# First batch of a fused attention and mixer kernel: half of x^T comes by scratch memory and VectorE's 32x32 transposes, and one half-batch of q, k and alpha is loaded later

## The chip, the core and the metric

The kernel runs on one core of one Trainium2 chip. The metric is the device time of one execution in microseconds; lower is better. TensorE (PE) multiplies matrices, VectorE (DVE), ScalarE (ACT) and GpSimd (POOL) work on elements, and SyncE (SP) issues nearly all DMAs. All engines run their own instruction streams and meet only at semaphores.

## The reference, cut to what matters

A gated linear attention over 4 batches, 8 heads, 768 tokens and head size 48 gives x; a token mixer and a channel mixer follow, and a last gated feed-forward layer.

```python
# attention, per batch and head
state = alpha[t][:, None] * state + outer(k[t], v[t])
y[t] = q[t] @ state                                  # x = y of all heads: (768 tokens, 384)
# token mixer and channel mixer
xt = x.transpose(0, 2, 1)
h = np.maximum(xt @ w_tok1, 0.0) @ w_tok2
u = x + h.transpose(0, 2, 1)
x2 = u + np.maximum(u @ w_ch1, 0.0) @ w_ch2
# gated feed-forward on x2 and its shifted copy (w_k, w_v, w_r)
```

The line that the change touches is `u = x + h^T`. The kernel keeps u with the 384 features on partitions, so it needs x^T, while the attention leaves x with the tokens on partitions.

## The kernel before

**Stages.** The program is one hand-written order for each engine. First comes the attention of batch 0 (the "head", `head_part`), in 24 steps: step i is token chunk c = i // 4 (128 tokens) and head pair p = i % 4. The loop runs over slots s = 0 to 27; in slot s the transposes and decay scans of step s run beside the scores of step s-2 and the outputs of step s-3. Then, for r = 1 to 3, the attention of batch r runs beside the mixer of batch r-1 (`batch_slot`, 28 slots each), then the mixer of batch 3 alone, then the feed-forward layer. From the end of the head on PE has matmuls of the mixer in every slot.

**Head, engine by engine.** In slot s ACT first copies the output of step s-3 out of PSUM (`high_x`: L953 to `x_sum`, L954 to `x_hi`), then spreads q of step s (`spread_q`, L975, semaphore `qbd_ready`), and then rounds half of one weight piece to `hi` (`split_half_hi`, L920): piece n is done in slots 3 + 2n and 4 + 2n, so piece 9 in slots 21 and 22. DVE does in each slot `mask`, `scans` (L1137, L1139), `scale_qk` (L1146 to L1154) and `outputs` (L1187, which waits for `xhi_ready` of step s-3). PE's scores of step i (L669, slot i+2) wait for `qbd_ready` of step i. POOL makes `x_lo` (`low_x`, semaphore `xlo_ready`) and the low part of each weight piece (semaphore `w_lo_ready`).

**Weights.** w_tok1, w_tok2, w_ch1 and w_ch2 are cut into 16 pieces of 384 KB, loaded one after the other into a ring of three buffers `w_raw`; pieces 0 to 9 are split in the head, piece 9 being the last of w_ch1; 10 to 15 are w_ch2. SP issues piece n once POOL has finished piece n-3. The slots in which SP comes to them: piece 9 in slot 16, piece 10 in 18, 11 in 20, 12 in 22.

**q, k, alpha and v of later batches.** `load_half(r, n)` loads 384 tokens of a head pair of batch r in 12 small DMAs (L367), `load_half_v(r, n)` the v beside them in 2 (L381). They fill `qka0`/`vt0` for even n and `qka1`/`vt1` for odd n. Steps 0 to 2 of batch 1 read half-batch (1, 0), steps 3 to 5 half-batch (1, 1); DVE's `turn` (L1124) of step 3 is in slot 4 of `batch_slot(1, ...)`.

**x^T.** For batches 1 to 3 x goes out to scratch memory (`store_x`), comes back in 32-row blocks (`load_x_blocks`, 4 DMAs for 128 features and 384 tokens) and is transposed by DVE in 32x32 blocks (`turn_x`, L1266); `down_base` then adds it to the token mixer's output (L1280). For batch 0 PE itself transposes x out of `x_sum` into the PSUM bank in which the token mixer's second product is then summed up (`token_down`, L767, `is_transpose`), and `down_base` only copies (L1275).

**After the head.** DVE does `split_low(1, 0)` (L1164, the low part of q of batch 1, step 0) and `tile_first(0, 0)`/`tile_second` (L1245, `h_lo`). PE claims a bank of `b_ring` for each tile of `token_down`, the first when `h_lo` has been read out of it (`tile_lo`). Token half 0 is tiles m = 0 to 2, half 1 the next three.

Of the kernel before, what the change touches and what calls it, by code (L numbers as in the profile page):

```python
# [13 lines left out]
def attention_mixer_channel_mix(nc, q, k, v, alpha, w_tok1, w_tok2, w_ch1, w_ch2,  # L14
# [39 lines left out]
    with ctx:  # L54
# [158 lines left out]
        x_raw_loaded = [sem(f"x_raw_loaded{n}") for n in range(2 * KC)]  # L213
        x_turned = sem("x_turned")
        x2_stored = [sem(f"x2_stored{n}") for n in range(2)]
        x2_loaded = [sem(f"x2_loaded{n}") for n in range(2)]
# [122 lines left out]
        def _(sp):  # L339
# [50 lines left out]
            def load_x_blocks(b, k):  # L390

                sp.wait_ge(x_rows_stored, 16 * (2 * KC * (b - 1) + k + 1))
                for a in range(4):
                    sp.dma_start(x_sum[32 * a:32 * (a + 1), k, :].rearrange("p (n j) -> p n j", j=32),
                                 x_rows[b][k].rearrange("(n p) (a j) -> a p n j", p=32, j=32)[a])\
                      .then_inc(x_raw_loaded[k], 16)

            def load_piece(n):
                dst, loaded, _ = staging(n)
# [21 lines left out]
            for s in range(SLOTS):  # L421

                if s % NP == 0 and 0 < s < NP * (NC - 2):
                    load_qka(s // NP + 2)
                if s % NP == 3 and 3 < s < NP * (NC - 2):
                    load_v(s // NP + 2)
                if s % NP == 0 and s >= NP * (NC - 2) and s < STEPS:
                    load_half(1, s // NP - NC + 2)
                if s % NP == 3 and s >= NP * (NC - 2) and s < STEPS:
                    load_half_v(1, s // NP - NC + 2)  # L430
                for n in pieces_in(s):
                    load_piece(n + NRAW)
            for n in range(2, 5):
                if n == 2:
# [195 lines left out]
        def _(pe):  # L630
# [131 lines left out]
            def token_down(b, half, m):  # L762
                t = KT + KC * half + m
                dst = claim(b, t)
                if b == 0:
                    for n in range(TM):
                        nc.tensor.matmul(dst[:, n * P:(n + 1) * P], x_sum[:, TM * half + n, m * P:(m + 1) * P],  # L767
                                         ident[:, :], start=(n == 0), stop=False, is_transpose=True)
                for n in range(3 * KT):
                    kt, (i, j) = n // 3, PASSES[n % 3]  # L770
                    if t == KT:
                        if i == 0:
                            pe.wait_ge(tile_hi, TILES * b + kt + 1)
                        else:
                            pe.wait_ge(tile_lo, TILES * b + kt + 3)
                    mm = nc.tensor.matmul(dst, h1[i][:, kt, m * P:(m + 1) * P], tok2_w(j, kt, half),  # L776
                                          start=(b > 0 and n == 0), stop=(n == 3 * KT - 1))
                mm.then_inc(tile_done, 1)
# [327 lines left out]
        def _(dve):  # L1106
# [143 lines left out]
            def read_sums(b, half):  # L1250

                for m in range(KC):
# [3 lines left out]
                                            ALU.add).then_inc(acc_read, 1)  # L1256

            def turn_x(b, k):

# [8 lines left out]
            def down_base(b, n):  # L1268
# [4 lines left out]
                dve.wait_ge(tile_done, TILES * b + t + 1)  # L1273
                if b == 0:
                    ins = nc.vector.tensor_copy(x2_half[half][:, m, :], src)  # L1275
# [56 lines left out]
            for s in range(SLOTS):  # L1332
                head_part(s)
            dve.wait_ge(mu_loaded, 32)
            nc.vector.tensor_scalar(omu[:, :, :], mu[:, :, :], -1.0, 1.0, ALU.mult, ALU.add).then_inc(omu_ready, 1)
# [74 lines left out]
```

## Time and profile before

| | |
|---|---|
| median of 3 runs | 732.37 us (732.33 to 732.41) |
| the profiled execution, its own time | 732.72 us |
| its span, first to last instruction | 731.0 us |
| PE busy | 725.3 us (99% of the span) |
| DVE busy | 472.0 us (65%) |
| ACT busy | 331.0 us (45%) |
| POOL busy | 197.1 us (27%) |
| granted clock of PE | 1.00 |

Times in the trace are counted from the start of the span. Some 1.7 us of an execution lie outside of the span. The clock of PE is granted in full in all 40 slices of the page. A busy share is an average over the whole program: the head, which ends at some 54 us, is limited by other things than the 670 us behind it.

### The profile page before, as it was taken

To read this page: it belongs to the slowest core of one execution; us is meant where nothing else is said; L and a number is where in the kernel's file an instruction comes from. 1 tells how busy PE (TensorE), PEld (TensorE's weight loads), DVE (VectorE), ACT (ScalarE), POOL (GpSimd) and SP (SyncE) were. 2 spreads that over 40 slices of the span, in tenths; PEclk is the share of its full clock that TensorE was granted. 3 is DMA by queue.
4 is the path that set the end of the run, shared out by engine and by line. 5 is a ranking of instruction groups with operands and counts; after the bars stand their busy time and mean duration, and the time that the engine had idled before them with its cause. 6 is when DMAs were issued, how large, how long until landed. Compare 5 with 4: busy or idle time off the path is not lost.

```text
span 731.0 us, 13851 instructions
## 1 busy us (share of the span) xinstructions
PE 725.3 (99%) x4556; PEld 719.3 (98%) x4556; DVE 472.0 (65%) x1297; ACT 331.0 (45%) x953; POOL 197.1 (27%) x344
## 2 busy tenths in 40 slices
PE   8999999999999999999999999999999999999998
PEld 8999999999999999999999999999999999999998
DVE  6988888865888875888883412446457375473561
ACT  4866544432544442444442332436346264373550
POOL 3875564333243331334432440310000000000000
PEclk9999999999999999999999999999999999999999
DMA  9973545542425544343531224010011010110000
GB/s 205 219 153 75 95 58 108 83 74 64 57 41 86 104 81 76 51 55 56 111 62 33 87 86 141 33 33 34 33 53 44 33 38 28 53 43 32 11 22 32
DMA packets 210043, 50.90 MB, mean 70 GB/s; under 512 B 190400, under 2 KB 207168, under 8 KB 209984
## 3 DMA queue, kind: packets, MB, share of 16 engines
q1 hardware_dynamic: 206992, 45.11, 31.1%
q0 software_dynamic: 1152, 4.72, 1.7%
q8 instruction: 29, 0.48, 0.3%
q10 hardware_dynamic: 1840, 0.34, 0.2%
q14 instruction: 30, 0.25, 0.1%
HBM read 37.17 MB, written 12.98 MB: 69 GB/s over the span
## 4 chain that ended last, share of the span: by engine, by line
PE 98%; DMA 1%; DVE 0%; issue 0%; ACT 0%; SPq 0%; DVEq 0%
PE bank L788 21%; PE bank L804 21%; PE bank L884 14%; PE bank L862 14%; PE bank L706 5%; PE bank L871 5%; PE bank L674 4%; PE bank L776 3%; PE bank L745 3%; PE bank L711 2%; PE bank L704 2%; PE bank L669 2%; PE bank L646 1%; PE bank L757 1%; PE bank L682 1%; PE bank L828 1%
## 5 line engine op out<-in xcount | busy, mean ns | idle before, releaser
L981 ACT ACTIVATE hid_hi<-bank 128x384 fp32r<-128x384 f32 x96 | 47.2, 492 | 115.5 <-PE bank L788 115.2
L1245 DVE SCALAR_TENSOR_TENSOR hid_lo<-bank,hid_hi 128x384 fp32r<-128x384 f32 x96 | 53.2, 555 | 65.5 <-ACT hid_hi L981 64.5
L1081 ACT ACTIVATE relu_k<-bank 128x384 f32<-128x384 f32 x64 | 31.5, 491 | 106.0 <-PE bank L862 86.2
L788 PE MATMUL bank<-u_hi,wch_hi 128*128 128x384 f32 x288 | 72.1, 358 | 0.0
L788 PE MATMUL bank<-u_lo,wch_hi 128*128 128x384 f32 x288 | 66.3, 338 | 0.0
L804 PE MATMUL bank<-hid_lo,wch_hi 128*128 128x384 f32 x288 | 65.5, 334 | 0.0
L788 PE MATMUL bank<-u_hi,wch_lo 128*128 128x384 f32 x288 | 65.5, 334 | 0.0
L804 PE MATMUL bank<-hid_hi,wch_hi 128*128 128x384 f32 x288 | 65.4, 334 | 0.0
L804 PE MATMUL bank<-hid_hi,wch_lo 128*128 128x384 f32 x288 | 65.4, 334 | 0.0
L1377 DVE TENSOR_TENSOR x_half<-bank,x_half 128x384 f32<-128x384 f32 x24 | 13.4, 558 | 77.4 <-PE bank L884 75.3
L557 POOL TENSOR_SCALAR_AFFINE_SELECT relu_k<-relu_k 128x256 f32<-128x256 f32 x72 | 29.3, 407 | 112.3 <-ACT relu_k L963 112.2
L954 ACT ACTIVATE x_hi<-bank 128x96 fp32r<-128x96 f32 x96 | 23.5, 245 | 78.1 <-PE bank L711 65.4
L1164 DVE SCALAR_TENSOR_TENSOR qs_lo<-qkd,rhead,qs_hi 96x128 fp32r<-96x128 f32 x144 | 50.8, 392 | 10.1 <-ACT qs_hi L975 9.3
L1363 DVE TENSOR_TENSOR relu_k<-relu_k 128x384 f32<-128x384 f32 x64 | 35.7, 558 | 27.8 <-ACT relu_k L1081 24.8
L788 PEld LDWEIGHTS bank<-u_lo,wch_hi 128*128 128x128 f32 x288 | 52.1, 188 | 0.0
L788 PEld LDWEIGHTS bank<-u_hi,wch_lo 128*128 128x128 f32 x288 | 51.5, 188 | 0.0
L804 PEld LDWEIGHTS bank<-hid_hi,wch_hi 128*128 128x128 f32 x288 | 51.2, 188 | 0.1
L804 PEld LDWEIGHTS bank<-hid_hi,wch_lo 128*128 128x128 f32 x288 | 51.3, 188 | 0.0
L804 PEld LDWEIGHTS bank<-hid_lo,wch_hi 128*128 128x128 f32 x288 | 51.3, 188 | 0.0
L562 POOL TENSOR_TENSOR ks_lo<-qkd,ks_hi 96x128 fp32r<-96x128 f32 x72 | 32.9, 457 | 62.5 <-ACT ks_hi L971 61.3
L706 PE MATMUL bank<-vt,relu_k 128*128 128x48 f32 x352 | 49.7, 264 | 0.0
L975 ACT ACTIVATE qs_hi<-qkd,rhead 96x128 fp32r<-96x128 f32 x144 | 49.0, 388 | 0.0
(141 smaller groups left out, 1833.6 us busy)
## 6 DMA issues: line engine op xcount, KB each, us to landing
w_raw<-in_moe_w_ch SPq DMA_DIRECT2D x12, 384.0 KB, 3.6
x_scratch<-x_half POOLq DMA_DIRECT2D x8, 576.0 KB, 3.6
out<-x_half SPq DMA_DIRECT2D x24, 192.0 KB, 1.9
vt<-in_v SPq DMA_DIRECT2D x48, 72.0 KB, 2.3
x_scratch<-x_sum SPq DMA_DIRECT2D x18, 192.0 KB, 2.1
x_sum<-x_scratch SPq DMA_DIRECT2D x72, 48.0 KB, 2.2
qka<-in_q SPq DMA_DIRECT2D x49, 48.0 KB, 2.2
qka<-in_alpha SPq DMA_DIRECT2D x49, 48.0 KB, 2.2
```

Source lines behind the costliest of these rows:

```text
L562: nc.gpsimd.tensor_tensor(ks[1][0:W2, i % 2, :], qkd[0:W2, second_of(i), :], ks[0][0:W2, i % 2, :], ALU.subtract)\
L706: mm = nc.tensor.matmul(y_ps[:, h * D:(h + 1) * D], am[:, i % 2, h * P:(h + 1) * P], v_of(r, i)[:, h * D:(h + 1) * D], start=(h == 0 and c ...
L788: mm = nc.tensor.matmul(dst, ch1_w(a, n % KC, jj), u[c][:, n % KC, half * HT:(half + 1) * HT], start=(n == 0), stop=(n == 3 * KC - 1))
L804: mm = nc.tensor.matmul(b_acc[m][:, 0:HT], ch2_w(a, jj, m), hid[c][:, j % HJ, :], start=(jj == 0 and n == 0), stop=(jj == NJ - 1 and n == 2))
L862: mm = nc.tensor.matmul(dst, wk_w(a, n % KC, j), mix_out[0][c][:, n % KC, :], start=(n == 0), stop=(n == 3 * KC - 1))
L871: mm = nc.tensor.matmul(b_acc[m][:, 0:DM], mix_out[1][a][:, n % KC, m * P:(m + 1) * P], wr_w(c, n % KC), start=(n == 0), stop=(n == 3 * KC ...
L884: mm = nc.tensor.matmul(bank[m][:, 0:DM], k2[a][:, n % NF, m * P:(m + 1) * P], wv_w(c, n % NF), start=(n == 0), stop=(n == 3 * NF - 1))
L975: nc.scalar.activation(dst[0:W2, h * P:(h + 1) * P], qkd[0:W2, first_of(i), :], ACT.Copy, scale=rhead[0:W2, i % 4, h:h + 1])\
L981: nc.scalar.activation(dst, b_ring[t % 2][:, 0:HT], func).then_inc(tile_hi, 1)
L1164: nc.vector.scalar_tensor_tensor(qs[1][0:W2, i % 2, cols], qkd[0:W2, first_of(i), :], rhead[0:W2, i % 4, h:h + 1], qs[0][0:W2, i % 2, cols ...
L1245: ins = nc.vector.scalar_tensor_tensor(dst, src, 0.0, hi, ALU.max, ALU.subtract)
L1363: nc.vector.tensor_tensor(relu_k[:, j % 2, :], relu_k[:, j % 2, :], relu_k[:, j % 2, :], ALU.mult).then_inc(k2_ready, 1)
```

## The change

For token half 0 of batch 0 (tokens 0 to 383) the way of the later batches is taken. SP stores these rows of `x_sum` to scratch memory in three DMAs (`store_first_x`, in slot 16, behind `load_half(1, 0)`), waits until they have landed and loads them back into `x_sum` in 12 DMAs (`load_first_x_blocks`, in slot 19, behind `load_half_v(1, 0)`). DVE transposes them into `x2_half[0]` in slots 25, 26 and 27 of the head (`turn_first_x`), and `down_base` adds that to the bank. PE's nine transposes of this half are gone; those of half 1 stay. `load_half(1, 1)` and `load_half_v(1, 1)`, which stood in slots 20 and 23, come after SP's loop over the slots.

```diff
+            def store_first_x():
+                sp.wait_ge(xlo_ready, NP * TM)
+                for m in range(KC):
+                    sp.dma_start(x_rows[0][m].rearrange("(c p) f -> p c f", p=P),
+                                 x_sum[:, 0:TM, m * P:(m + 1) * P]).then_inc(first_rows_stored, 16)
+
+            def load_first_x_blocks():
+                sp.wait_ge(first_rows_stored, 16 * KC)
+                for m in range(KC):
+                    for a in range(4):
+                        sp.dma_start(x_sum[32 * a:32 * (a + 1), m, :].rearrange("p (n j) -> p n j", j=32),
+                                     x_rows[0][m].rearrange("(n p) (a j) -> a p n j", p=32, j=32)[a])\
+                          .then_inc(first_raw_loaded[m], 16)
...
-                if s % NP == 0 and s >= NP * (NC - 2) and s < STEPS:
-                    load_half(1, s // NP - NC + 2)
-                if s % NP == 3 and s >= NP * (NC - 2) and s < STEPS:
-                    load_half_v(1, s // NP - NC + 2)
+                if s == NP * (NC - 2):
+                    load_half(1, 0)
+                    store_first_x()
+                if s == NP * (NC - 2) + 3:
+                    load_half_v(1, 0)
+                    load_first_x_blocks()
                 for n in pieces_in(s):
                     load_piece(n + NRAW)
+            load_half(1, 1)
+            load_half_v(1, 1)
...
-                if b == 0:
+                turned_by_pe = b == 0 and half == 1
+                if turned_by_pe:
                     for n in range(TM):
                         nc.tensor.matmul(dst[:, n * P:(n + 1) * P], x_sum[:, TM * half + n, m * P:(m + 1) * P],
                                          ident[:, :], start=(n == 0), stop=False, is_transpose=True)
...
+            def turn_first_x(m):
+                dve.wait_ge(first_raw_loaded[m], 64)
+                nc.vector.transpose(x2_half[0][:, m, :], x_sum[:, m, :]).then_inc(first_turned, 1)
...
-                if b == 0:
+                if b == 0 and half == 0:
+                    dve.wait_ge(first_turned, m + 1)
+                    ins = nc.vector.tensor_tensor(x2_half[0][:, m, :], src, x2_half[0][:, m, :], ALU.add)
+                elif b == 0:
                     ins = nc.vector.tensor_copy(x2_half[half][:, m, :], src)
...
             for s in range(SLOTS):
                 head_part(s)
+                if STEPS + 1 <= s <= STEPS + KC:
+                    turn_first_x(s - STEPS - 1)
```

SP's stream from the end of `load_half(1, 0)` (slot 16) on, before. `qka0` is the buffer of half-batch (1, 0), `qka1` that of (1, 1), `w_ch1` is piece 9, the `w_ch2` rows are pieces 10, 11, 12 and 13:

```order
L367 DMA qka0<-in_alpha 32x12x32
L404 DMA w_raw<-in_moe_w_ch1 128x768
L404 DMA w_raw<-in_moe_w_ch2 128x2x384
L381 DMA vt0<-in_v 128x3x48 x2
L367 DMA qka1<-in_q 32x12x32
...
L367 DMA qka1<-in_alpha 32x12x32
L404 DMA w_raw<-in_moe_w_ch2 128x2x384 x2
L381 DMA vt1<-in_v 128x3x48 x2
L404 DMA w_raw<-in_moe_w_ch2 128x2x384
```

The same place of the changed kernel (its own line numbers):

```order
L370 DMA qka0<-in_alpha 32x12x32
L405 DMA x2_scratch<-x_sum 128x3x128 x3
L422 DMA w_raw<-in_moe_w_ch1 128x768
L422 DMA w_raw<-in_moe_w_ch2 128x2x384
L384 DMA vt0<-in_v 128x3x48 x2
L412 DMA x_sum<-x2_scratch 32x12x32 x12
L422 DMA w_raw<-in_moe_w_ch2 128x2x384 x2
L370 DMA qka1<-in_q 32x12x32
...
L370 DMA qka1<-in_alpha 32x12x32
L384 DMA vt1<-in_v 128x3x48 x2
L422 DMA w_raw<-in_moe_w_ch2 128x2x384
```

Three stores now stand ahead of piece 9, and twelve block loads take the place of the twelve loads of half-batch (1, 1), which come behind pieces 11 and 12.

DVE's stream at the end of the head and the start of batch 1, of the changed kernel, from the last instruction of `scale_qk(1, 0)` on:

```order
L1177 TENSOR_TENSOR qkd<-bank,decays 96x2x128 [waits scores_done,suffix_ready]
L1284 STREAM_TRANSPOSE x_half<-x_sum 128x384 [waits first_raw_loaded0]
L1284 STREAM_TRANSPOSE x_half<-x_sum 128x384 [waits first_raw_loaded1]
L1284 STREAM_TRANSPOSE x_half<-x_sum 128x384 [waits first_raw_loaded2]
L1368 TENSOR_SCALAR omu<-mu 128x6 [waits mu_loaded]
L1187 SCALAR_TENSOR_TENSOR qs_lo<-qkd,rhead,qs_hi 96x128 [waits qbd_ready,rhead_ready]
L1187 SCALAR_TENSOR_TENSOR qs_lo<-qkd,rhead,qs_hi 96x128 [waits qbd_ready]
L1268 SCALAR_TENSOR_TENSOR h_lo<-bank,h_hi 128x384 [waits tile_hi] x2
```

The three transposes are new; the other rows stood one behind the other before. `split_low(1, 0)` and `h_lo` are now queued behind the last of the twelve block loads.

## Rows read from the trace of the kernel before

**Rows 1.** The page, busy time of each engine.

```profile
PE 725.3 (99%) x4556; PEld 719.3 (98%) x4556; DVE 472.0 (65%) x1297; ACT 331.0 (45%) x953; POOL 197.1 (27%) x344
```

**Rows 2.** ACT in order of time, 45.5 to 48.3 us; in brackets idle time before.

```profile
46.31 0.53 ACT L920 ACTIVATE wch_hi<-w_raw 128x384 fp32r<-128x384 f32 x1 [0.37 <-DMA w_raw<-in_moe_w_ch]
...
46.87 0.24 ACT L954 ACTIVATE x_hi<-bank 128x96 fp32r<-128x96 f32 x1
47.08 0.69 ACT L975 ACTIVATE x_half<-qkd,rhead 96x128 f32<-96x128 f32 x2
```

**Rows 3.** DVE in order of time, 46 to 49 us.

```profile
47.15 0.31 DVE L1187 SCALAR_TENSOR_TENSOR state<-state,decays,bank 96x96 f32<-96x96 f32 x1
```

**Rows 4.** PE in order of time, 46 to 49 us: start, us, engine, line, work.

```profile
47.92 0.67 PE L669 MATMUL bank<-x_half,qkd 96*128 96x256 f32 x2
```

**Rows 5.** SP's DMA issues in order of time, 24 to 80 us.

```profile
40.70 2.30 SPq L367 DMA_DIRECT2D qka<-in_alpha  x4
43.04 0.94 SPq L404 DMA_DIRECT2D w_raw<-in_moe_w_ch  x2
44.03 1.00 SPq L381 DMA_DIRECT2D vt<-in_v  x2
45.08 2.10 SPq L367 DMA_DIRECT2D qka<-in_q  x4
...
52.13 0.98 SPq L404 DMA_DIRECT2D w_raw<-in_moe_w_ch  x2
```

**Rows 6.** PE in order of time, 56 to 64 us.

```profile
56.10 0.52 PE L767 MATMUL bank<-ident,x_sum 128*128 128x128 f32 x3 [0.29 <-DVE h_lo L1245]
...
59.51 0.49 PE L767 MATMUL bank<-ident,x_sum 128*128 128x128 f32 x3
...
62.29 0.28 PE L674 MATMUL bank<-qs_hi,ks_hi 96*128 96x256 f32 x1
```

**Rows 7.** PE in order of time, 177 to 180 us, token mixer of batch 1.

```profile
177.64 0.42 PE L776 MATMUL bank<-wtok_hi,h_hi 128*128 128x384 f32 x1
...
179.81 0.28 PE L674 MATMUL bank<-qs_hi,ks_hi 96*128 96x256 f32 x1
```

**Rows 8.** Line L767, PE's transposes.

```profile
L767 PE MATMUL bank<-ident,x_sum x18: 270/272/300, 56.1 to 64.3; 128*128 128x128 f32 x18
```

**Rows 9.** Lines L1275 and L1280, down_base.

```profile
L1275 DVE COPY x_half<-bank x6: 557/557/558, 57.7 to 65.7; 128x384 f32<-128x384 f32 x6
...
L1280 DVE TENSOR_TENSOR x_half<-bank,x_half x9: 520/558/559, 176.3 to 412.5; 128x384 f32<-128x384 f32 x9
```

**Rows 10.** Line L1266, DVE's transposes of x of later batches.

```profile
L1266 DVE STREAM_TRANSPOSE x_half<-x_sum x9: 567/568/570, 128.3 to 410.0; 128x384 f32<-128x384 f32 x9
```

**Rows 11.** DVE in order of time, 51 to 68 us.

```profile
51.53 0.41 DVE L1154 TENSOR_TENSOR qkd<-bank,decays 96x256 f32<-96x256 f32 x1
...
54.10 0.71 DVE L1164 SCALAR_TENSOR_TENSOR qs_lo<-qkd,rhead,qs_hi 96x128 fp32r<-96x128 f32 x2 [2.08 <-ACT qs_hi L975]
55.40 1.09 DVE L1245 SCALAR_TENSOR_TENSOR h_lo<-bank,h_hi 128x384 fp32r<-128x384 f32 x2 [0.59 <-ACT h_hi L981]
...
67.05 0.58 DVE L1124 STREAM_TRANSPOSE bank<-qka 96x384 f32<-96x384 f32 x1
```

**Rows 12.** Line L387, the stores of x of later batches.

```profile
L387 SPq DMA_DIRECT2D x_scratch<-x_sum x18: 383/384/432, 102.3 to 399.6; - x18
```

**Rows 13.** DMAs issued from 43.0 to 43.4 us: KB each, us to landing.

```profile
w_raw<-in_moe_w_ch SPq DMA_DIRECT2D x1, 384.0 KB, 3.2
```

**Rows 14.** Windows: PE, PEld, DVE, ACT, POOL busy, PE's clock, DMA share, GB/s.

```profile
103.00:104.00 1.00, 1.00 (x9) 1.00 (x9) 1.00 (x3) 0.64 (x3) 0.65 (x2) 1.00 0.79 212
```

**Rows 15.** Line L912, ACT's splits of pieces 10 to 12.

```profile
L912 ACT ACTIVATE wch_hi<-w_raw x3: 829/838/849, 56.3 to 68.5; 128x768 fp32r<-128x768 f32 x3
```

**Rows 16.** The page, DMA issues: KB each, median us to landing.

```profile
x_scratch<-x_sum SPq DMA_DIRECT2D x18, 192.0 KB, 2.1
x_sum<-x_scratch SPq DMA_DIRECT2D x72, 48.0 KB, 2.2
```

More of the change, by code:

```diff
@@ L214, in attention_mixer_channel_mix @@
         x_turned = sem("x_turned")
+        first_rows_stored = sem("first_rows_stored")
+        first_raw_loaded = [sem(f"first_raw_loaded{n}") for n in range(KC)]
+        first_turned = sem("first_turned")
         x2_stored = [sem(f"x2_stored{n}") for n in range(2)]
@@ L776, in token_down @@
                     mm = nc.tensor.matmul(dst, h1[i][:, kt, m * P:(m + 1) * P], tok2_w(j, kt, half),
-                                          start=(b > 0 and n == 0), stop=(n == 3 * KT - 1))
+                                          start=(n == 0 and not turned_by_pe), stop=(n == 3 * KT - 1))
                 mm.then_inc(tile_done, 1)
```

## The prediction, on record before the changed kernel ran

> **What bounds the kernel now.** I read the page first: PE is busy for 725.3 of 731.0 us [rows 1], so whatever PE loses or wins between the head and the end stays in the time; no later stage has an idle PE that could absorb it. The head is the exception: there PE, DVE and ACT pass the same step around, so I read it in order of time at 46 to 49 us, where the change puts its DMAs. ACT splits the first half of weight piece 9 at 46.31, after 0.37 us of waiting for its DMA [rows 2]: already now this piece comes late. DVE's state update L1187 at 47.15 [rows 3] comes right behind the copy `x_hi` that ACT finishes at 46.87 + 0.24 = 47.11 [rows 2]. PE's scores at 47.92 [rows 4] come right behind `spread_q`, finished at 47.08 + 0.69 = 47.77 [rows 2]. In this place ACT thus has no slack towards either of them. SP is the third thing to see: it issues without a break from 40.70 on, about 0.5 us for each DMA, and so it is late against its slots [rows 5]. Piece 9 is issued at 43.04 because that is when SP gets there.
>
> **Removed: nine transposes of PE.** Two tiles with transposes take from 59.51 to 62.29, 2.78 us [rows 6]; two tiles of batch 1 without them, from 177.64 to 179.81, 2.17 us [rows 7]. So a tile gets 0.305 us cheaper, and three **0.9 us**. A transposing instruction is listed with 272 ns [rows 8], but it overlaps its neighbours; 9 x 0.272 = 2.45 us is the upper end, nothing (if PE then waited for a bank) the lower. I take 0.9, because the difference of two pitches counts what the queue sees. PE has no wait inside these tiles behind the first one, at 56.10 [rows 6].
>
> The Trainium skill, "TensorE: Matmul & The Clock Gate", Part 4, gives about 275 ns for a PE transpose in a kernel's context. The rows agree with this as a duration (272 ns), not as a pitch; by that rule the change would win 2.5 us here in place of 0.9. That is rival 3 below.
>
> **Added on DVE: three block transposes and an add for a copy.** The add from PSUM takes 558 ns, as the copy does with 557 [rows 9]: nothing. The transposes take 0.57 us each [rows 10]. Their place is behind `scale_qk(1, 0)`, which ends at 51.53 + 0.41 = 51.94; DVE then idles 2.08 us until 54.10 [rows 11], which holds all three, 1.7 us. They cost nothing unless their blocks are late, which is the second wait below; without this cover they would cost up to 1.7.
>
> **Added on SP, the first wait: piece 9.** The three stores stand ahead of piece 9. The wait in front of them, for `xlo_ready` of step 11 (slot 14), is over: ACT is in slot 21 at 46.31 [rows 2]. Issue takes 0.384 us each [rows 12] and some 0.05 between, together 1.3 us, so piece 9 is issued at 44.35 in place of 43.04. It landed 3.2 us after its issue [rows 13]; with nothing else this gives a delay of 1.3, the lower end. But the stores also bring 3 x 196.6 = 590 kB. A stretch with such a store moved 212 GB/s with 0.79 of the DMA engines busy [rows 14], so 268 GB/s when full: 590 kB take 2.2 us. If the piece waits for all of it, the delay is 2.2. With issue stalls on a full queue (the twelve DMAs from 45.08 to 52.13 took 7.05 us, where 12 x 0.515 = 6.2 would do [rows 5]) I put the upper end at 2.6. I take **1.9**, nearer the full transfer, since the stores' bytes go first.
>
> "DMA: Bandwidth & Descriptors", Queues, rings and completion order, in the Trainium skill says that each DMA engine consumes the descriptors of a ring in order. No row here shows two such DMAs apart; by that rule alone the delay would be 2.2.
>
> What is queued behind: ACT waits at the split of piece 9 in slot 21, and `x_hi` of step 19 and `spread_q` of step 22 stand behind it. DVE's L1187 and PE's L669 follow directly, so the head from 46.3 on moves by the same 1.9. Neither can work ahead: DVE's next mask and scans stand behind L1187, PE's outputs and token products behind L669. From 48 us on PE has no idle time in which to make it up. Pieces 10 to 12 are also later, but ACT splits them from 56.3 to 68.5 only [rows 15].
>
> **Added on SP, the second wait: the blocks.** The last store is issued at about 43.9. One lands after 2.1 us alone [rows 16]; three in a row should land by 46.9. SP meanwhile issues two pieces (0.98) and v (1.00) [rows 5] and is there at 46.4. The twelve block loads take 6.2 to 7.05 us, so the last is issued at 52.6 to 53.5 and lands 2.2 later [rows 16], at 54.8 to 55.7; call it T, 55.3. DVE then needs 0.57 for the last transpose, the small `omu` and 0.71 for `split_low`, so `h_lo` can begin at T + 1.3 = 56.6. Before it began at 55.40 [rows 11]; with the head moved by 1.9 it is due at 57.3. So the second wait is hidden behind the first by some 0.7 us and adds nothing. Were the first gone, it would cost 56.6 - 55.4 = 1.2 by itself. The two don't add up: PE loses the larger.
>
> **Moved: half-batch (1, 1).** Twelve loads and two of v go past twelve block loads and pieces 11 and 12. After the blocks (53.1 to 54.0) and the pieces (0.98) they start at 54.1 to 55.0, take up to 7.05 and land by 64.3. DVE's `turn` of step 3 reads them at 67.05 [rows 11], about 1 us later with the shift. At least 2.7 us are left: nothing. Pieces 11 and 12, issued now at 52.13 [rows 5], come 1 to 2 us later, and ACT comes to them long behind piece 10: nothing. Piece 13 waits for POOL anyway.
>
> **Sum.** +1.9 (piece 9) + 0 (blocks, hidden) - 0.9 (transposes) = +1.0 us on a span of 731.0, so 732.0; with the 1.7 us outside of it the profiled execution would take 733.7, against 732.72 before. The median of the runs is 0.35 lower than that execution: 732.37 + 1.0 = 733.4.
>
> **The rivals.** A measurement of this kernel can tell about 0.2% from no change, 1.46 us, so bounds are 730.9 and 733.8.
>
> Forecast, chance 0.68: delays of 1.3 to 2.6 for piece 9, less 0.9, is +0.4 to +1.7: 732.8 to 734.1. About a third of it is over 733.8.
>
> Rival 1, slower, 0.12: the blocks are late after all. SP would have to lose 2 us more, as when one issue takes over 1.7 us because the DMA queue is full (the stores, two pieces and v are about 1.5 MB within 3 us), or the stores' landing is late. It decides once T is later than 56.0; at T = 57.4, PE loses 3.3 and wins 0.9: +2.4, 734.8. For it speaks the stretch from 45.08, 0.9 us slower than its issue pitch; against it that this 0.9 is already in my 53.5.
>
> Rival 2, no change, 0.08: piece 9 is not held up, since stores and loads overlap and its landing was long only because of its neighbours. Then the blocks alone cost 1.2: +0.3, 732.7.
>
> Rival 3, a little faster, 0.05: the transposes give back their whole 2.45 us. 1.9 - 2.45 = -0.55: 731.8.
>
> Rival 4, faster, 0.07: neither wait reaches PE, since the head has slack that I don't see. -0.9 gives 731.5, and with the full price of the transposes -2.45, 729.9; about half of it passes the bound.
>
> **How the numbers follow.** The predicted time is the forecast's, 733.4. The range has to reach from rivals 2 to 1; 731.9 to 735.0 leaves out rivals 3 and 4 and the late end of rival 1, together under 2 in 10. Slower by over 0.2%: 0.22 of the forecast and all of rival 1, 0.34. Faster: 0.06 from rivals 3 and 4. The rest, 0.60, is within 0.2%.
>
> **What would show it.** In the profile after: three stores of x from about 43.0 and piece 9 at 44.3; ACT idle about 2.2 us before a split L-line of `wch_hi`, released by the DMA into `w_raw`, where 0.37 stood; PE idle for about 1.9 us before its scores at some 49.8. The three block transposes of DVE around 54 to 56, the last with a wait for its DMA, and no wait of `split_low` that names them. The first token product about 1.9 us later than 56.1, and three tiles of 1.1 us in place of 1.4. SP's loads for `qka1` from about 54.5, with no wait for them at DVE's `turn`. The step most likely wrong is the delay of piece 9: if ACT's wait there is under 1.3 or over 2.6, my DMA argument fails. If PE idles for a second time before its first token product, it is the blocks.

## The result: 0.65% slower, 5.5 us where 1.0 was forecast

| | before | changed |
|---|---|---|
| median | 732.43 us (732.33 to 732.94, 6 runs) | 737.94 us (736.05 to 739.61, 6 runs) |
| the profiled execution | 732.72 us | 737.68 us |
| its span | 731.0 us | 736.0 us |
| mean granted clock, each run | 1.0 | 0.998; 0.995 three times; 0.993 twice |

The ratio is 1.0065 with a 95% interval of 1.0038 to 1.0091: slower, and above the predicted range of 731.9 to 735.0. The runs of the changed kernel spread over 3.6 us where those of before spread over 0.6, and they go with the clock: 736.05 at 0.998, three at 737.6 to 738.2 and 0.995, the two above 739 at 0.993. The two medians alone would give a ratio of 1.0075. Each experiment below has its ratio to the kernel before on its own chip.

The page of the changed kernel, engines and granted clock:

```profile
PE 727.7 (99%) x4547; PEld 721.5 (98%) x4547; DVE 473.1 (64%) x1300; ACT 331.0 (45%) x953; POOL 197.2 (27%) x344
...
PEclk9998999999999999999999999999999999999999
```

PE has nine instructions fewer and is nevertheless 2.4 us longer busy than in [rows 1]. The fourth slice of the clock, from 55 us on, is lower than the others. Busy time that grows while work shrinks is the first sign that a wait is not all that was added.

**The first wait.** A DMA is issued when SP hands it over, and lands when its data is there and its semaphore says so. SP's stream in the timeline (start, duration to the last of a group, line, count):

```profile
42.42 1.56 SPq L405 DMA_DIRECT2D x_scratch<-x_sum  x3
44.02 1.22 SPq L422 DMA_DIRECT2D w_raw<-in_moe_w_ch  x2
45.29 1.05 SPq L384 DMA_DIRECT2D vt<-in_v  x2
46.68 7.41 SPq L412 DMA_DIRECT2D x_sum<-x_scratch  x12
54.13 0.98 SPq L422 DMA_DIRECT2D w_raw<-in_moe_w_ch  x2
55.16 1.99 SPq L370 DMA_DIRECT2D qka<-in_q  x4
```

Piece 9 is issued at 44.02. The head runs 0.35 us ahead of the execution of before in this one, so against the work around it the issue is 0.98 + 0.35 = 1.33 us later than the 43.04 of [rows 5]. That is the 1.3 worked out, with some luck: the three stores took 1.60 us of SP, and the alpha loads ahead of them 0.30 less than before (2.00 for 2.30). How long it took to land, from the DMA view of 44.0 to 44.5 us (last column: us from issue to landing):

```profile
w_raw<-in_moe_w_ch SPq DMA_DIRECT2D x1, 384.0 KB, 5.1
```

It was 3.2 us in [rows 13]. To the start of ACT's split it is 5.08 now and was 3.27. ACT in the timeline:

```profile
49.10 0.52 ACT L943 ACTIVATE wch_hi<-w_raw 128x384 fp32r<-128x384 f32 x1 [3.51 <-DMA w_raw<-in_moe_w_ch]
...
49.66 0.24 ACT L977 ACTIVATE x_hi<-bank 128x96 fp32r<-128x96 f32 x1
49.80 0.68 ACT L998 ACTIVATE x_half<-qkd,rhead 96x128 f32<-96x128 f32 x2
```

Where ACT waited 0.37 us in [rows 2] it waits 3.51: 3.14 more, 1.33 of it from the issue and 1.81 from the landing. `x_hi` and `spread_q` follow at once, as they did before. PE's timeline shows the gap, and three places by which to measure what is behind it:

```profile
50.62 0.67 PE L691 MATMUL bank<-x_half,qkd 96*128 96x256 f32 x2 [2.99 <-DVE relu_k L1194]
...
60.97 0.28 PE L696 MATMUL bank<-qs_hi,ks_hi 96*128 96x256 f32 x1
...
61.83 0.41 PE L799 MATMUL bank<-wtok_hi,h_hi 128*128 128x384 f32 x1 [0.26 <-issue]
...
70.26 0.36 PE L726 MATMUL bank<-state,qkd 96*128 96x96 f32 x2
```

The first are the scores that stood at 47.92 [rows 4]: +2.70. The second are the scores of batch 1, step 0; the last the first state product of batch 1 behind the tiles of the token mixer. The two in the kernel before:

```profile
55.21 0.28 PE L674 MATMUL bank<-qs_hi,ks_hi 96*128 96x256 f32 x1
...
65.48 0.36 PE L704 MATMUL bank<-state,qkd 96*128 96x96 f32 x2
```

From the first place to the second it is 7.29 us before and 10.35 now: **3.06 us more, with not one instruction more and no new wait of that size**. From the second to the third it is 10.27 before and 9.29 now: the transposes give back 0.98. 2.70 + 3.06 - 0.98 = 4.8 of the 5.0 by which the spans differ.

**The clock.** The busy times by windows of 2 us tell where the 3.06 are:

```profile
core 0: us, PE busy (x) PEld busy (x) DVE busy (x) ACT busy (x) POOL busy (x), PEclk, DMA share, GB/s
...
48.00:50.00 2.00, 0.00 (x0) 0.00 (x0) 0.06 (x1) 0.90 (x4) 0.02 (x1) 1.00 0.89 182
50.00:52.00 2.00, 1.38 (x10) 1.35 (x11) 1.96 (x8) 1.26 (x6) 1.74 (x3) 1.00 0.50 80
52.00:54.00 2.00, 2.00 (x8) 1.91 (x7) 1.44 (x4) 0.86 (x4) 1.49 (x3) 0.56 0.57 92
54.00:56.00 2.00, 2.00 (x9) 1.91 (x9) 1.46 (x6) 0.39 (x2) 0.00 (x0) 0.50 0.70 116
56.00:58.00 2.00, 2.00 (x10) 2.00 (x8) 1.04 (x4) 0.00 (x0) 0.39 (x1) 0.50 0.99 340
58.00:60.00 2.00, 2.00 (x11) 2.00 (x11) 0.24 (x1) 1.17 (x5) 0.75 (x2) 0.73 0.96 121
60.00:62.00 2.00, 1.74 (x12) 1.57 (x11) 1.30 (x4) 1.32 (x4) 0.07 (x1) 1.00 0.58 70
```

PE stands still through 48 to 50, resumes at full clock, and from 52 on is granted 0.50, that is 1.2 GHz in place of 2.4. In "2.00 busy" it now completes 8 to 11 instructions, and the others wait for it. One minus the granted clock, times 2 us, summed over the rows, estimates the time that the clock took: 0.88 + 1.00 + 1.00 + 0.54 = 3.4 us. I call this the clock's share below. It is a little too high, since the two places above are only 3.06 us further apart.

**The blocks.** DVE in the timeline:

```profile
55.50 1.48 DVE L1284 STREAM_TRANSPOSE x_half<-x_sum 128x384 f32<-128x384 f32 x3
...
59.76 0.72 DVE L1187 SCALAR_TENSOR_TENSOR qs_lo<-qkd,rhead,qs_hi 96x128 fp32r<-96x128 f32 x2 [2.72 <-ACT qs_hi L998]
```

The three transposes run without a wait (the last block was issued at 53.62 and landed 2.0 us later, at 55.6), and `split_low` behind them waits for ACT, not for a block. The slow clock had a part in that: DVE came to them late, behind a wait of 1.04 us (at 54.51) for PE's slowed scores.

### The profile page after: what moved, and what is told of

It reads as the page before. It is cut to its first block, busy times and chain, and to the rows that moved or that the text cites. A ratio compares the mean times of both kernels' runs of the same rounds, so it can differ in the third digit from the quotient of the medians.

```text
span 736.0 us, 13854 instructions
## 1 busy us (share of the span) xinstructions
PE 727.7 (99%) x4547; PEld 721.5 (98%) x4547; DVE 473.1 (64%) x1300; ACT 331.0 (45%) x953; POOL 197.2 (27%) x344
## 4 chain that ended last, share of the span: by engine, by line
PE 93%; DVE 4%; DMA 1%; issue 1%; POOL 0%; ACT 0%; SPq 0%; DVEq 0%; POOLq 0%
PE bank L811 21%; PE bank L827 20%; PE bank L907 14%; PE bank L885 14%; PE bank L894 5%; PE bank L728 4%; PE bank L696 4%; PE bank L799 3%; PE bank L767 3%; PE bank L726 2%; PE bank L733 2%; DVE relu_k L1194 1%; PE bank L779 1%; DVE decays L1160 1%; DVE decays L1162 1%
## 5 line engine op out<-in xcount | busy, mean ns | idle before, releaser
L1187 DVE SCALAR_TENSOR_TENSOR qs_lo<-qkd,rhead,qs_hi 96x128 fp32r<-96x128 f32 x144 | 51.0, 393 | 10.6 <-ACT qs_hi L998 9.7
```

What stands on the lines that cost most here:

```text
L1187: nc.vector.scalar_tensor_tensor(qs[1][0:W2, i % 2, cols], qkd[0:W2, first_of(i), :], rhead[0:W2, i % 4, h:h + 1], qs[0][0:W2, i % 2, cols ...
```

## The experiments

The theory after the result: piece 9 is held up by the sum of issue and bytes, and the gap that this opens in PE's stream brings the clock down. The rival within it: the clock falls for another reason (the blocks, the new order, the slower DVE), and would fall without the gap. The other rival: it is the wait for the blocks that costs.

### The stores alone, and with an eighth of their bytes

`stores only` is the kernel before with the three stores and SP's wait for their landing; `small stores` writes 16 of the 128 partitions. Nothing else of the change is in them.

```diff
+                if s == NP * (NC - 2):
+                    store_first_x()
                 if s % NP == 3 and s >= NP * (NC - 2) and s < STEPS:
                     load_half_v(1, s // NP - NC + 2)
+                if s == NP * (NC - 2) + 3:
+                    sp.wait_ge(first_rows_stored, 16 * KC)
...
+                    sp.dma_start(x_rows[0][m].rearrange("(c p) f -> p c f", p=P)[0:16],   # small stores
+                                 x_sum[0:16, 0:TM, m * P:(m + 1) * P]).then_inc(first_rows_stored, 16)
```

> The kernel before with nothing but the three stores of x ahead of weight piece 9 (and the wait for their landing in slot 19). The output is the reference's; no block loads, no block transposes, PE keeps all its transposes. Theory A (the stores hold up piece 9, ACT waits, PE's gap lets the clock fall): ACT waits about 3.5 us for the piece, PE idles about 3 us at 47.5, the granted clock is 0.5 to 0.6 for some 6 us behind it, and the time is that of the changed kernel plus the 0.9 us of the transposes, 737 to 740. Rival B (the blocks or the moved half-batch do the damage): 732 to 733.5 with a clock of 1.00.

> As e1_stores_only, but each store takes 16 of the 128 partitions, an eighth of the bytes (only that part of scratch memory is written, and nothing reads it). If the bytes hold up piece 9: it lands about 1 us later than before (issue time of three DMAs), ACT waits about 1.3 us, no fall of the clock, 733 to 734. If it is the number of DMAs in the queue whatever their size: as e1, ACT waits 3 us or more.

Measured: stores only 738.94 us (737.06 to 741.13, 7 runs), ratio 1.0076 [1.0054, 1.0098]; small stores 737.65 (733.57 to 741.22, 10 runs), 1.0046 [1.0015, 1.0078]. ACT in the timeline of stores only, and then of small stores:

```profile
49.89 0.52 ACT L931 ACTIVATE wch_hi<-w_raw 128x384 fp32r<-128x384 f32 x1 [4.10 <-DMA w_raw<-in_moe_w_ch]
```

```profile
48.35 0.52 ACT L931 ACTIVATE wch_hi<-w_raw 128x384 fp32r<-128x384 f32 x1 [2.83 <-DMA w_raw<-in_moe_w_ch]
```

Three stores do it all; x^T, the blocks and the moved half-batch are not needed for the loss. The piece was issued at the same time in both (44.35 and 44.37) and ACT's split began 5.54 and 3.98 us later: seven eighths of the bytes are about 1.6 us, in one profiled execution each. So the bytes count on top of the issue. But I expected small stores at 733 to 734 with a wait of 1.3, and it missed: ACT waited 2.46 us more than before. Against the work around it the piece was issued 1.75 us late, not 1.0, and it landed 0.7 us more slowly than in the kernel before. PE's row in small stores, and the window of 48 to 50 us:

```profile
49.87 1.19 PE L680 MATMUL bank<-x_half,qkd 96*128 96x256 f32 x2 [2.31 <-DVE relu_k L1182]
```

```profile
48.00:50.00 2.00, 0.13 (x1) 0.16 (x1) 0.81 (x3) 1.65 (x6) 0.73 (x2) 0.82 1.02 259
```

A gap of 2.31 us, and the clock took 3.4. Here it had fallen before PE came back: the window has 0.82 although PE stood still for nearly all of it, and the first scores take 1.19 us where 0.67 is usual.

### The gap filled with idle products

The changed kernel, with 16 products of the identity that nobody reads ahead of PE's slot 24. The kernel before already has such products (`keep_warm`) in its first slots.

```diff
             for s in range(SLOTS):
+                if s == STEPS:
+                    keep_warm(16)
                 head_part(s)
```

> The changed kernel with 16 matmuls of the identity, whose result nobody reads, in PE's stream ahead of slot 24, where it idled 3.0 us. Theory A: PE's next scores still start at about 50.6, the clock stays at 1.00, and the time is 3 us less, 734.5 to 735.5, with no more spread than before. If the clock falls by itself, or for another reason than the gap, it falls here too and the time stays at 736 to 739.6 or rises by the 16 matmuls.

Measured: 735.21 us (734.84 to 736.17, 10 runs), ratio 1.0032 [1.0020, 1.0044], the mean clock 1.0 in every run. PE in the timeline (each product is listed as two instructions):

```profile
47.20 3.80 PE L851 MATMUL bank<-ident 128*128 128x128 f32 x32
50.86 0.67 PE L691 MATMUL bank<-x_half,qkd 96*128 96x256 f32 x2
```

and the windows behind:

```profile
52.00:54.00 2.00, 2.00 (x15) 1.93 (x15) 1.88 (x6) 0.96 (x4) 1.73 (x3) 1.00 0.60 95
54.00:56.00 2.00, 2.00 (x16) 2.00 (x16) 1.77 (x6) 0.39 (x2) 0.40 (x1) 1.00 0.57 92
```

ACT's wait was even longer here, 4.02 us, and the scores no earlier (50.86). Yet 15 and 16 instructions fit where 8 and 9 did, at clock 1.00. 2.7 us are gone (2.4 by the ratios, which compare each kernel with its own chip) and most of the spread: 1.3 us are left of 3.6. The blocks, the order and DVE's work are the same as in the changed kernel, so the rival on the clock falls: it comes down because PE stood still. What is left, 2.1 us of span, is 2.94 of delay less 0.98 of transposes, and that is the mechanism that was forecast, at a larger size. The blocks are no longer hidden, though. DVE reaches its transposes at 54.78, and the third waits:

```profile
57.14 0.58 DVE L1286 STREAM_TRANSPOSE x_half<-x_sum 128x384 f32<-128x384 f32 x1 [1.34 <-DMA x_sum<-x_scratch]
```

PE then idles 0.26 us before the scores of batch 1.

### The late piece without stores

The kernel before, where SP waits ahead of piece 9 for a semaphore that is due at some time: `y_done` of 19 (held mid), `tr_done` of 23 (held long), `xlo_ready` of 19 (held short). No byte is added. The cut shows held mid.

```diff
                 for n in pieces_in(s):
+                    if n + NRAW == 9:
+                        sp.wait_ge(y_done, 19)
                     load_piece(n + NRAW)
```

> The kernel before, in which SP also waits for x_lo of step 18 (about 43.7) before it issues piece 9: the piece is issued some 0.6 us later and no byte or DMA is added. ACT's wait goes from 0.4 to about 1.0 us, PE gets a gap of about 0.6 us, the clock holds, and the time is 732.8 to 733.5. If any wait at this place lets the clock fall: 735 or more.

> As e11, but SP waits for the transposes of step 22 (about 45.1): piece 9 is issued some 2 us later, again with nothing added. Theory A (what hurts is only how late the piece is, and then PE's gap and clock): ACT waits 2.5 to 3.5 us, PE idles 2 to 3 us, the granted clock falls to 0.5 for some microseconds, 736 to 740 as the changed kernel and e1. If the fall of the clock needed the stores' traffic: 734.5 to 735.5 with a clock of 1.00.

> The kernel before, in which SP also waits for the outputs of step 18 (about 44.0) before it issues piece 9, so that it is issued some 1.1 us later with nothing added: between the kernel before (no gap of PE) and e12 (2.3 us). ACT waits about 1.5 us and PE idles about 1.1 us. If a gap of this size costs only itself, 733.3 to 734.3 with a clock of 1.00; if the clock falls as behind the longer gaps, 735.5 to 739 with a wide spread.

Measured: held short 738.48 (737.97 to 740.58, 4 runs), 1.0083 [1.0062, 1.0104]; held long 736.53 (734.92 to 739.83, 6), 1.0061 [1.0038, 1.0085]; held mid 736.65 (733.41 to 739.68, 10), 1.0050 [1.0029, 1.0071]. Held short was misnamed: its semaphore came late, the piece was issued at 46.56, and PE's gap was 3.53 us. As a small dose it failed; as a large one it shows that a late piece without any store costs as much as the change. ACT and PE of held mid:

```profile
48.85 0.52 ACT L922 ACTIVATE wch_hi<-w_raw 128x384 fp32r<-128x384 f32 x1 [3.12 <-DMA w_raw<-in_moe_w_ch]
```

```profile
50.37 0.89 PE L671 MATMUL bank<-x_half,qkd 96*128 96x256 f32 x2 [2.61 <-DVE relu_k L1173]
```

Here the piece was issued at 43.99, 0.95 late (1.17 against the work around it), and no store stood in the queue ahead of it; with a landing of 3.2 us it would have cost some 1.2. It took 4.8. The DMA view of 46.7 to 46.9 us shows a packet of another queue at that time (packets, MB, share of 16 engines):

```profile
q8 instruction: 1, 0.02, 29.2%
```

0.2 us x 16 x 0.292 is 0.93 us of one DMA engine, and such a fetch of instructions comes every 12 to 21 us in the first 130 us of the kernel before. It starts at 47.0 in the kernel before, when piece 9 has landed (46.3); at 46.2 in the changed kernel, while the piece is on its way. Held short has no such packet between the piece's issue and its landing, and landing took 3.2; in held long it starts at 45.1, when the piece has just been issued and its data does not move yet (no traffic from 45.25 to 46.0), and landing took 3.4. That the packet holds up a late piece is read from traces and not shown: no run varied it by itself, its 0.93 us are less than the 1.6 by which held mid's landing is longer, and in small stores and stores first (below) the piece also met one and landed 4.0 us after its issue. Three of the ten runs of held mid took 733.41 to 733.73 at mean clock 1.0, about 1 us above the kernel before (732.60 on that chip). It may be that the piece landed in the usual time there; they have no profile. So the dose that held mid was meant to give, a gap of 1.1 us, was not measured.

### Stores at other places

The changed kernel with the stores ahead of `load_half(1, 0)` (stores first), or right behind piece 9 (stores later), or with piece 9 issued behind the q loads of half-batch (1, 0) (piece 9 first).

```diff
                 if s == NP * (NC - 2):
+                    store_first_x()              # stores first
                     load_half(1, 0)
-                    store_first_x()
...
                 for n in pieces_in(s):
                     load_piece(n + NRAW)
+                if s == NP * (NC - 2):           # stores later
+                    store_first_x()
...
                 for a, t in enumerate((q, k, alpha)):
+                    if a == 1 and inside is not None:    # piece 9 first: load_half(1, 0, 9)
+                        load_piece(inside)
```

> The changed kernel with the three stores ahead of the 12 loads of half-batch (1, 0) in place of behind them: piece 9 is issued as late (about 44.1), but the bytes of the stores have been moved by then. If the bytes count: piece 9 lands after about 3.3 us at 47.4, ACT waits 1.5 to 2 us, PE idles 1 to 1.5 us; if the clock holds over that the time is 732.4 + 1.2 - 0.9, 732.5 to 733.5. If the issue alone counts: as the changed kernel, 736 to 740.

> The changed kernel with the three stores behind piece 9 in place of ahead of it. Piece 9 is issued at 43.0 and lands within 3.3 us, ACT waits 0.3 to 0.6 us, no gap at 47.5. The blocks are as late as in the changed kernel or later, last landing 55.6 to 57.5, and now stand alone: PE idles 1.5 to 4 us ahead of its first token product and the clock may fall there: 734 to 738. If only the first wait mattered: 731.5 to 732.5.

> The changed kernel with one DMA moved: weight piece 9 is issued behind the four q loads of half-batch (1, 0), at about 38.5, in place of behind alpha and the stores at 44.0. Theory A: ACT no longer waits at its split, PE has no gap at 47.5. What is left is the wait for the blocks: their last lands at about 55.6, as in the changed kernel, so h_lo starts near 57 where 55 would be due, PE idles 1.5 to 2.5 us ahead of its first token product, and 0.9 comes back from the transposes: 733 to 734 if the clock holds, 736 or more if this gap lets it fall too. If the blocks were hidden by more than the first wait: 731.5.

Measured: stores first 737.69 (735.86 to 739.24, 7 runs), 1.0051 [1.0033, 1.0069]; stores later 737.49 (736.54 to 738.89, 4), 1.0068 [1.0051, 1.0085]; piece 9 first 736.72 (733.88 to 737.69, 9 runs; a tenth took 883.67 and is left out), 1.0039 [1.0013, 1.0065]. Stores first was expected at 732.5 to 733.5 if the bytes count, and missed that: the piece was issued at 45.04 and not at 44.1, 1.8 us late against the work around it, and landed in 4.0 us, 1.1 less than in the changed kernel but 0.7 more than in the kernel before. PE had a gap of 2.38 us. So it does not part issue and bytes as it was meant to. PE of stores later:

```profile
48.07 0.67 PE L692 MATMUL bank<-x_half,qkd 96*128 96x256 f32 x2 [0.40 <-DVE relu_k L1195]
...
59.31 0.36 PE L697 MATMUL bank<-qs_hi,ks_hi 96*128 96x256 f32 x1 [3.82 <-DVE qs_lo L1188]
```

and DVE and PE of piece 9 first:

```profile
57.58 0.58 DVE L1287 STREAM_TRANSPOSE x_half<-x_sum 128x384 f32<-128x384 f32 x1 [2.44 <-DMA x_sum<-x_scratch]
```

```profile
58.98 0.55 PE L699 MATMUL bank<-qs_hi,ks_hi 96*128 96x256 f32 x1 [4.03 <-DVE qs_lo L1190]
```

Both take the first gap of PE away or nearly so and run into the second: DVE now waits for the blocks (57.58 and 57.91), PE idles 4.03 and 3.82 us before the scores of batch 1, and then the clock falls, with a share of 3.4 in piece 9 first and 1.7 in stores later. A gap of 0.40 left it at 1.00.

### Merged block loads, same place

The changed kernel with the three stores cut by token chunk and the 12 block loads as 4 of 144 KB; the blocks are all there when the last has landed.

```diff
-                for m in range(KC):
-                    for a in range(4):
-                        sp.dma_start(x_sum[32 * a:32 * (a + 1), m, :].rearrange("p (n j) -> p n j", j=32),
-                                     x_rows[0][m].rearrange("(n p) (a j) -> a p n j", p=32, j=32)[a])\
-                          .then_inc(first_raw_loaded[m], 16)
+                for a in range(4):
+                    sp.dma_start(x_sum[32 * a:32 * (a + 1), 0:KC, :].rearrange("p m (n j) -> p (m n) j", j=32),
+                                 blocks3[a]).then_inc(first_raw_loaded[0], 16)
```

> The changed kernel with nothing but its twelve block loads made four. Piece 9 still stands behind the stores, issued at 44.0. Theory A: ACT's wait of 3 us, PE's gap and the fall of the clock stay, since they come ahead of the blocks: 736 to 740 as the changed kernel. If the blocks had a part in the loss: under 735.

Measured: 738.87 us (737.49 to 740.49, 4 runs), 1.0069 [1.0047, 1.0090]; ACT's wait 3.61, PE's gap 3.09. Cheaper block loads take nothing off the loss of the changed kernel, and stores only has the loss without any.

### One account for nine kernels

For the profiled execution of each kernel in which piece 9 is late: PE's gap before the scores, how much later than 47.92 they start, the clock's share by the windows, the transposes (0.98 where they are gone), the sum, and the span less 731.0.

| kernel | gap | later | clock | transposes | sum | span |
|---|---|---|---|---|---|---|
| changed | 2.99 | 2.70 | 3.4 | -0.98 | 5.1 | 5.0 |
| stores only | 3.59 | 3.49 | 1.7 | | 5.2 | 5.1 |
| small stores | 2.31 | 1.95 | 3.4 | | 5.4 | 4.9 |
| gap filled | none | 2.94 | 0 | -0.98 | 2.0 | 2.1 |
| stores first | 2.38 | 2.65 | 5.1 | -0.98 | 6.8 | 6.5 |
| merged, same place | 3.09 | 3.53 | 5.1 | -0.98 | 7.7 | 7.3 |
| held short | 3.53 | 3.34 | 3.4 | | 6.7 | 6.1 |
| held long | 2.27 | 2.13 | 1.7 | | 3.8 | 3.7 |
| held mid | 2.61 | 2.45 | 1.7 | | 4.2 | 4.0 |

Two terms, delay and clock, and the transposes where they are gone, give all nine within 0.6 us. These are single executions, and some lie over a microsecond off the median of their kernel (stores only 737.82 against 738.94).

### The half-batch alone, and both waits taken away

Four kernels: the kernel before with only half-batch (1, 1) moved behind the loop (move only); the kernel before with piece 9 behind the q loads (before, piece 9 first); the changed kernel with the stores first, piece 9 behind the q loads and the blocks right behind `load_half(1, 0)` (early all); and that with the merged block loads (merged early).

```diff
                 if s == NP * (NC - 2):
-                    load_half(1, 0)
                     store_first_x()
+                    load_half(1, 0, 9)
+                    load_first_x_blocks()
                 if s == NP * (NC - 2) + 3:
                     load_half_v(1, 0)
-                    load_first_x_blocks()
```

> The kernel before with only half-batch (1, 1) moved behind SP's loop over the slots. Theory A: its loads land by 60 to 62, DVE's turn of step 3 reads them at 67, no wait appears: 732.4 to 733, no difference. If the move does harm: DVE waits for qka1 and the time rises by over 1 us.

> The kernel before with piece 9 issued behind the four q loads of half-batch (1, 0). Theory A, if the piece is late already now: ACT's wait of 0.37 us goes, the median falls by 0.1 to 0.4 us to 732.1 to 732.6, and the single executions of 733.5 to 740 that the kernel before shows on this chip (7 of 25) disappear, since a pause in SP's issue no longer reaches ACT. If those executions have another cause they stay.

> The changed kernel with SP's order in slot 16: three stores, q loads, piece 9, k and alpha loads, then the twelve block loads; piece 10 and v behind them. Piece 9 is issued at about 40.5, the last block lands at 53.5 to 55. Theory A: no wait of ACT for piece 9, no or under 0.5 us of wait for the blocks, clock 1.00, and the 0.9 us of the transposes are seen at last: 731.3 to 732.0, faster than before by about 0.1%. If the transposes on PE are worth nothing, or the extra DMAs cost something else: 732.4 or more.

> As e6_early_all, but the twelve block loads of 48 KB are four of 144 KB. If SP's issue costs about 0.5 us for each DMA whatever its size, SP is 4 us earlier from 47 us on: the last block lands by 50.5 to 52, DVE does not wait for it, the loads of half-batch (1, 1) land by 60, no wait is left of those that e6 had (0.28 us of PE, 0.47 us of DVE), and the median is 731.2 to 731.8 with a spread under 1 us. If issue goes by the number of 128-byte runs, it is as e6: 732.5 with single executions up to 735.

| kernel | us | ratio |
|---|---|---|
| move only | 732.45 (732.22 to 733.11, 10 runs) | 0.9986 [0.9962, 1.0010] |
| before, piece 9 first | 732.46 (732.24 to 732.96, 12) | 0.9985 [0.9964, 1.0005] |
| early all | 732.47 (731.41 to 734.97, 12) | 0.9982 [0.9958, 1.0006] |
| merged early | 732.03 (731.69 to 732.76, 11) | 0.9980 [0.9971, 0.9990] |

The move costs nothing. Ahead of piece 9, 0.37 us of waiting was all there was to win in the kernel before, and it can't be told from nothing. None of the 12 runs of this kernel was over 733; of 34 of the kernel before on the same chip 3 were over 738, which is too few to say that the early piece removed them. Early all was expected at 731.3 to 732.0 and missed; it has still a wait of 0.28 on PE and a wide spread. Merged early, DVE, SP and PE:

```profile
53.07 1.50 DVE L1287 STREAM_TRANSPOSE x_half<-x_sum 128x384 f32<-128x384 f32 x3 [1.06 <-DMA x_sum<-x_scratch]
```

```profile
46.04 3.82 SPq L415 DMA_DIRECT2D x_sum<-x_scratch  x4
```

```profile
55.39 0.36 PE L699 MATMUL bank<-qs_hi,ks_hi 96*128 96x256 f32 x1
```

The blocks cost SP 3.8 us in place of the 6.9 of early all, less of a saving than the 4 expected, and the last landed at 53.0, not by 50.5 to 52. DVE's wait is over in time, and PE goes on without one. In the profiled executions early all and merged early have spans of 730.1 and 730.2 against 731.0; but move only and the kernel before with piece 9 first have 730.6, so that only 0.4 to 0.9 us of it can be put down to the change. The median of merged early, outside of the expected 731.2 to 731.8, is 0.4 us under that of the kernel before with the result (732.43) and 1.6 under the 733.63 of that kernel on its own chip, where the kernel before itself was higher than elsewhere; the interval excludes 1, but I would count on some 0.5 us, not on 1.6.

## Why the prediction was wrong

**Where it would happen: right.** Three stores ahead of piece 9, ACT's wait at the split, DVE's L1187 and PE's L669 behind it, nothing in the stages behind to make it up. Stores only and the three held kernels show this chain by itself.

**The first failed step: "I take 1.9, nearer the full transfer", with 2.6 as upper end.** Measured in the profiled execution: 3.14 us on ACT and 3.05 on PE's scores (2.70 + 0.35). By its own sign, a wait over 2.6, the DMA argument failed. I took a value between 1.3 of issue and 2.2 of bytes, as if both ran from the same moment. The piece is issued 1.33 later, and then takes 1.81 longer to land. A plain sum, 1.3 + 2.2 = 3.5, would have been a safer upper end, though stores only passes even that (3.73). The bytes are part of the 1.81: small stores puts seven eighths of them at 1.6. They are not shown to be all of it: held mid shows 1.6 without any bytes, from another cause, and stores first and small stores 0.7 with none or an eighth of them ahead. How these share it in the changed kernel is open. The prediction also put long issues of SP down to a full queue; no run shows that.

The rule of the Trainium skill, "DMA: Bandwidth & Descriptors", Queues, rings and completion order, that a ring's descriptors are consumed in order, fits the bytes ahead being paid for, which the 1.6 us between stores only and small stores bear out. By that rule alone I had given 2.2; the trace has 3.14, so it is not the whole account.

**The second failed step, and the one that puts the time outside the range: the sum "+1.9 (piece 9) + 0 (blocks, hidden) - 0.9 (transposes)" has no term for the clock, 3.06 us.** It took a wait at its length. The gap filled with products shows that the fall of the clock behind it is worth 2.7 us of 5.5 and most of the spread. Nothing in the profile before could give the price, since PE has no such gap in this place, but the prediction should have asked what PE does after standing still for two microseconds, and named it as a rival. The code gave a hint: `keep_warm` spends PE's time on products that nobody reads.

**The blocks: right here with help, wrong alone.** T was 55.3 (54.8 to 55.7), measured 55.6. They were hidden behind the first wait, as said, but also behind the slow clock: where the clock held, in the gap filled, DVE waited 1.34 us for the last block (at 57.1) and PE idled 0.26. "Were the first gone, it would cost 1.2 by itself" failed: piece 9 first and stores later have 4.03 and 3.82 us of gap there, and the clock on top. The loads came later than worked out (the last landed at 57.6 and 57.9), as SP could start on them only at 48.9 and 49.3: the stores landed late, and the issue of v took 2.4 us in place of 1.0. So rival 1's mechanism is real and stands right behind the first.

**The transposes: right.** 0.9 forecast, 0.98 measured, and this is the pitch of the queue. The same stretch has 10.24 to 10.28 us in all eight kernels with the transposes, and 9.28 in stores first and in merged, same place. Rival 3, the whole 2.45 us, is refuted; so is the figure of the Trainium skill ("TensorE: Matmul & The Clock Gate", Part 4) when taken as what a removed transpose gives back: it is a duration (given for bf16; here, in fp32, 272 ns), and nine of them gave 0.11 us each.

**The moved half-batch, DVE's three transposes and the add: right,** nothing each. The half-batch was issued from 55.16 (54.1 to 55.0 foreseen), no wait names it, and move only shows no difference.

**Rivals 2 and 4,** that the piece would not be held up or that neither wait would reach PE, are refuted by the 3.51 us and the gap of 2.99. With the right size of the delay, 3.1, the forecast would have read +2.2, 734.6, within the range; only the clock's share put the time outside it. The gap filled is the measured form of this: 2.5 us above the kernel before on its chip. The weakest number was thus not the one that I called weakest, but one that wasn't there.

**Open:** why the clock's share is 1.7 in one execution and 3.4 or 5.1 in another of about the same gap; what the shortest gap is that lets the clock fall, as no profile has one between 0.40 and 2.27 us; and how much of the late landing is the instruction packet.

## What to carry to other kernels

Where PE is 99% busy, price a new gap at its length plus what the clock takes behind it, and look at both in the windows; a gap that can't be avoided may be filled with idle products, which here gave back half of the loss. DMAs put ahead of one that somebody waits for cost it their issue and much of the time of their bytes on top, and two waits in a row hide each other: mend both before you judge the idea. Look at the order of the issues first and at their number next: with piece 9 and the blocks moved forward the loss was gone (732.47), and four loads in place of twelve made a small gain of that (732.03), where the same four loads in the old place helped nothing (738.87).

## What the runs showed that I had not expected

- Behind a gap of PE of 2.3 to 4.0 us at this place, the granted clock went to 0.50 (1.2 GHz) in every profiled execution; behind gaps of 0.28 and 0.40 it stayed at 1.00. In the changed kernel PE first ran on at full clock, from 50.6 to some 52.3; in small stores and held short the clock had fallen when PE came back (first scores 1.19 us in place of 0.67). Not every execution shows a fall: one run each of small stores (733.57), held long (734.92) and piece 9 first (733.88), and three of held mid, have a mean clock of 1.0. They have no profile.
- The kernel before has such executions too: on the chip of stores only 3 of 25 (736.55, 737.31 and 739.90, mean clock 0.998, 0.997 and 0.993), on that of piece 9 first 3 of 34 (738.32 to 740.23). With ACT already waiting 0.37 us for piece 9 it may take only one slow DMA; none of them was profiled.
- The share that it took does not grow with the gap, but comes in three sizes: 1.7, 3.4 and 5.1 us (stores only 1.7 at a gap of 3.59, stores first 5.1 at 2.38). The six runs of the changed kernel have the same pattern, 736.05, 737.6 to 738.2, 739.3 to 739.6.
- One instruction fetch of 16 KB every 12 to 21 us takes 0.9 us or more of one DMA engine, and transfers in flight with it landed 4.0 (small stores) to 4.8 us (held mid) after their issue where 3.2 is usual; that it is the cause is not shown. At about the same time one issue of SP often takes 1.2 to 2.0 us in place of 0.5.
- SP's issue costs about 0.5 us for 24 KB and for 384 KB alike, but the merged block loads of 144 KB took 0.8 us each (median). Why is open.
